# First layer by Strassen's seven products on three 768-token tiles, in a kernel of windowed attention and two MLPs

## The reference

```
c: chunk of 32 queries; its keys are 8 memory keys + 16 before + 32 + 8 after     (8 heads of 64)
x = softmax(q k^T / 8) v                          # 3072 x 512
h = max(x @ w1, x @ w2, x @ w3);  y = h @ w_out   # MLP 1: 512 -> 768 (three times) -> 512
u = y @ w_in2                                     # MLP 2: 512 -> 2048
g = u if u >= 1, 0 if u <= -1, else (u + 1)^2 / 4
out = g @ w_out2                                  # 2048 -> 512
```

## Time and profile before

| | |
|---|---|
| median of 3 runs | 984.15 us (984.12 to 984.52) |
| the profiled execution | 983.69 us |
| its span, first to last instruction | 981.6 us |
| TensorE busy | 968.8 us |
| VectorE, ScalarE, GpSimd busy | 469.6, 354.5, 150.0 us |
| moved by DMA | 181.52 MB, mean 185 GB/s |

### The profile page before, as it was taken

The page is one execution under the profiler, slowest core; times in us unless marked ns, Lnnn a source line. Parts: engine busy times, 40 slices in busy tenths (PEclk is TensorE's granted clock), DMA queues, the critical chain, the costliest instruction groups (busy, mean ns, idle before and its releaser), DMA issues.

```text
span 981.6 us, 18566 instructions
## 1 busy us (share of the span) xinstructions
PE 968.8 (99%) x7968; PEld 905.1 (92%) x7968; DVE 469.6 (48%) x713; ACT 354.5 (36%) x553; POOL 150.0 (15%) x176
## 2 busy tenths in 40 slices
PE   6999999999999999999999999999999999999998
PEld 5999999999999999999998888988888888888887
DVE  4662524244252434425456655566545666454452
ACT  3342212222222222222353625545354544444253
POOL 2022442405235230000000000000000000000000
PEclk9999999999999999999999999999999999999999
DMA  9462753645465361042735566655756545575532
GB/s 363 186 234 70 267 183 128 252 144 188 162 236 183 153 231 61 1 172 65 269 131 217 203 220 215 204 196 200 249 191 236 192 161 196 187 258 170 198 118 108
DMA packets 32206, 181.52 MB, mean 185 GB/s; under 512 B 3456, under 2 KB 7552, under 8 KB 21888
## 3 DMA queue, kind: packets, MB, share of 16 engines
q0 software_dynamic: 9216, 92.28, 27.0%
q1 hardware_dynamic: 22912, 88.09, 24.4%
HBM read 144.70 MB, written 35.65 MB: 184 GB/s over the span
## 4 chain that ended last, share of the span: by engine, by line
PE 98%; DMA 1%; DVE 0%; ACT 0%; issue 0%; SPq 0%
PE mlp_ps L491 23%; PE mlp_ps L492 23%; PE mlp_ps L493 23%; PE attn_ps L493 3%; PE scores_ps L493 3%; PE attn_ps L492 3%; PE scores_ps L492 3%; PE attn_ps L491 3%; PE scores_ps L491 3%; PE attn_ps L484 3%; PE scores_ps L457 2%; PE trans_ps L493 2%; PE trans_ps L492 2%; PE trans_ps L491 1%; PE trans_ps L466 1%; DMA qk_raw<-qk_l 1%
## 5 line engine op out<-in xcount | busy, mean ns | idle before, releaser
L491 PE MATMUL mlp_ps<-x_hi,w_hi 128*128 128x384 f32 x572 | 195.1, 341 | 0.0
L493 PE MATMUL mlp_ps<-x_lo,w_hi 128*128 128x384 f32 x572 | 191.5, 335 | 0.0
L492 PE MATMUL mlp_ps<-x_hi,w_lo 128*128 128x384 f32 x572 | 191.2, 334 | 0.0
L492 PE MATMUL mlp_ps<-yc,wi 128*128 128x384 f32 x448 | 150.7, 336 | 0.0
L493 PE MATMUL mlp_ps<-yc,wi 128*128 128x384 f32 x448 | 149.6, 334 | 0.0
L491 PE MATMUL mlp_ps<-yc,wi 128*128 128x384 f32 x448 | 149.6, 334 | 0.0
L787 ACT ACTIVATE ramp<-up,half_col 128x768 f32<-128x768 f32 x64 | 60.1, 939 | 197.4 <-DVE up L1004 178.2
L491 PEld LDWEIGHTS mlp_ps<-x_hi,w_hi 128*128 128x128 f32 x572 | 107.4, 188 | 1.9
L492 PEld LDWEIGHTS mlp_ps<-x_hi,w_lo 128*128 128x128 f32 x572 | 107.5, 188 | 0.0
L493 PEld LDWEIGHTS mlp_ps<-x_lo,w_hi 128*128 128x128 f32 x572 | 107.4, 188 | 0.0
L492 PEld LDWEIGHTS mlp_ps<-yc,wi 128*128 128x128 f32 x448 | 84.1, 188 | 8.8
(11 more groups left out here) (138 smaller groups left out, 1653.0 us busy)
## 6 DMA issues: line engine op xcount, KB each, us to landing
wi<-wi_scratch POOLq DMA_DIRECT2D x32, 1792.0 KB, 7.5
wo<-wo_scratch POOLq DMA_DIRECT2D x32, 1024.0 KB, 5.1
qk_raw<-qk_l SPq DMA_DIRECT2D x24, 768.0 KB, 8.1
wi_scratch<-stage_a SPq DMA_DIRECT2D x8, 1792.0 KB, 8.2
v_raw<-v_l SPq DMA_DIRECT2D x24, 512.0 KB, 4.8
wo_scratch<-stage_a SPq DMA_DIRECT2D x8, 1024.0 KB, 6.6
y_scratch<-y_stage SPq DMA_DIRECT2D x32, 192.0 KB, 2.6
y_raw<-y_scratch SPq DMA_DIRECT2D x8, 768.0 KB, 5.3
```

Of the source, the lines that this page charges most:

```text
L491: pe.matmul(out_ap, a_hi, b_hi, start=first, stop=False, skip_group_check=beside)
L492: pe.matmul(out_ap, a_lo, b_hi, start=False, stop=False, skip_group_check=beside)
L493: return pe.matmul(out_ap, a_hi, b_lo, start=False, stop=last, skip_group_check=beside)
```

## The change

MLP 1 keeps two tiles of 384 tokens (`first_tile`, `second_tile`; the second carries six groups of attention). The other 2304 tokens go through three tiles of 768 (`strassen_tile`, v = 0, 1, 2). In each, the six column blocks and three matrices make nine pairs of column blocks (`PAIRS_S = 9`), 27 in all, and each is made with seven products over 2 x 2 blocks, in a form with partial sums that are added up in PSUM: products 0, 2, 4 and 6 use one bank without clearing it, 3 and 5 another. ScalarE copies the bank after products 0, 2, 3 and 4 (`snapshot`), VectorE adds products 1 and 5 and the copy of 3 (`block_sum`), and takes the maximum over the three matrices (`block_max`). Attention of the next tile, six groups, is spread over the 63 product slots, one group in ten slots; tile 2 has none. Layer 2 of a tile is eight products (`l2_product`).

The left operands are made by GpSimd: an item is a pair, made in two halves (`split_half`), stored to `wi_scratch` by GpSimd's own queue and streamed back for each pair with `load_wi` into two buffers. There are 17 items (9 of MLP 1, 8 of MLP 2). Fourteen halves (`AHEAD`) are made during the two plain tiles, the first five (`EARLY`) with one staging buffer and the rest with two; the others are made one per pair. The right operands `yc1` are made from `x_raw` at each tile's start (`xc_sum`, `xc_high`, `xc_low`). `load_wi(0)` waits for the end of the second tile's layer 1.

MLP 2 uses the same scheme of products: five copies by ScalarE and three folds by VectorE in a period. Its output weights are no longer stored split; GpSimd loads them raw each period (512 KB for 1024) and splits them (`split_wo`).

```diff
-PRODUCTS = (("m1", 0, P, 4), ("m2", 3 * P, 2 * P, 5), ("m5", 2 * P, 2 * P, 6), ("m3", 10 * P, P, 1),
-            ("m4", 12 * P, P, 0), ("m7", 8 * P, P, 3), ("m6", 6 * P, P, 2))
+PAIRS_S = 3 * KFP
+EARLY, AHEAD = 5, 14
+PRODUCTS = ((W_A11, Y_B11), (W_A12, Y_B21), (W_S2, Y_T2), (W_S1, Y_T1), (W_S3, Y_T3), (W_S4, Y_B22), (W_A22, Y_T4))
...
# GpSimd
+            def split_half(n):
+                raw = w_raw[:, n % 2]
+                sums, both = staging(n)
...
+                pool.wait_ge(raw_in[n % 2], 16 * (n // 2 + 1))
...
+                pool.tensor_tensor(s3, a11, a21, ALU.subtract).then_inc(w_sums_done, 1)
+                pool.tensor_tensor(s1, a21, a22, ALU.add).then_inc(w_sums_done, 1)
+                pool.tensor_tensor(s2, s1, a11, ALU.subtract).then_inc(w_sums_done, 1)
+                pool.tensor_tensor(s4, a12, s2, ALU.subtract).then_inc(w_sums_done, 1)
+                if n >= EARLY + 2:
+                    pool.wait_ge(w_stored[n % 2], 16 * (n // 2))
+                elif 0 < n < EARLY:
+                    pool.wait_ge(w_stored[(n - 1) % 2], 16 * ((n - 1) // 2 + 1))
+                pool.tensor_copy(hi[:, 0:4 * P], raw).then_inc(w_hi_done, 1)
+                pool.tensor_copy(hi[:, 4 * P:7 * P], sums).then_inc(w_hi_done, 1)
+                pool.tensor_tensor(lo[:, 0:4 * P], raw, hi[:, 0:4 * P].bitcast(F32), ALU.subtract).then_inc(w_split, 1)
+                pool.tensor_tensor(lo[:, 4 * P:7 * P], sums, hi[:, 4 * P:7 * P].bitcast(F32), ALU.subtract).then_inc(w_split, 1)
...
+                pool.dma_start(wi_scratch[n // 2][:, n % 2 * W_COLS:(n % 2 + 1) * W_COLS], both).then_inc(w_stored[n % 2], 16)
+                if n + 2 < 2 * ITEMS:
+                    load_raw(n + 2)
...
+            load_raw(0)
+            load_raw(1)
+            for n in range(AHEAD):
+                split_half(n)
+            pool.wait_ge(mlp_done, TG + L1G)
+            load_wi(0)
+            load_wi(1)
+            for g in range(PERIODS_S):
+                if AHEAD + g < 2 * ITEMS:
+                    split_half(AHEAD + g)
+                pool.wait_ge(l1_done, 7 * (g + 1))
+                load_wi(g + 2)
...
+            for g in range(PERIODS):
+                split_wo(g)
+                if g + 1 < PERIODS:
+                    pool.wait_ge(wo_split, 2 * (g + 1))
+                    load_wo(g + 1)
+                if g + 2 < PERIODS:
+                    pool.wait_ge(prod_done, 7 * (g + 1))
+                    load_wi(PERIODS_S + g + 2)
# TensorE
+            def l1_product(g, i):
+                v, q = divmod(g, PAIRS_S)
+                if i == 0:
+                    pe.wait_ge(wi_in[g % 2], 16 * (g // 2 + 1))
+                    if q == 0:
+                        pe.wait_ge(x_split, 8 * (v + 1))
+                if i < 2 and q == 0:
+                    pe.wait_ge(y_copied, y_before(v) - 1 + i)
+                elif i < 2:
+                    pe.wait_ge(summed, 3 * g - 2 + 2 * i)
+                elif i == 3:
+                    if q and (q - 1) % 3:
+                        pe.wait_ge(merged, merges(g - 1) + 4)
+                    elif q:
+                        pe.wait_ge(c21_copied, (g - 1) // 3 + 1)
+                else:
+                    pe.wait_ge(snapped, 4 * g + (0, 0, 1, 0, 2, 3, 4)[i])
+                wcols, ycols = (slice(n * c, (n + 1) * c) for n, c in zip(PRODUCTS[i], (P, TT)))
+                w, x = wi[g % 2], yc1
+                begins = i in (0, 1, 3)
+                for j in range(2):
+                    last = three(l1_bank(g, i), (w[:, j, 0, wcols], w[:, j, 1, wcols], x[:, j, 0, ycols], x[:, j, 1, ycols]),
+                                 begins and j == 0, j == 1, not begins)
+                last.then_inc(l1_done, 1)
# ScalarE
+            def snapshot(g, i):
+                act.wait_ge(l1_done, 7 * g + i + 1)
...
+                copy(snap[:, f, t], l1_bank(g, i)).then_inc(snapped, 1)
# VectorE
+                dve.tensor_tensor(to[:, f, t], snap[:, f, t], other, ALU.add).then_inc(summed, 1)
...
+                dve.tensor_tensor(h_run[:, f, t], h_run[:, f, t], other, ALU.max).then_inc(merged, 1)
...
+            def xc_low(v, j, k):
+                dve.wait_ge(xc_hi_done, 4 * (2 * v + j) + HI_ORDER.index(k) + 1)
+                hi, lo = (yc1[:, j, i, Y_PARTS[k]] for i in range(2))
+                dve.tensor_tensor(lo, xc_source(j, k), hi.bitcast(F32), ALU.subtract).then_inc(x_split, 1)
```

More of the change, by code:

```diff
@@ L517, in layer1 @@
                 for k in range(KD):
-                    if ahead is not None and k == KD - 1:
+                    if ahead is not None and k == at:
                         ahead()
@@ L564, in tile_a @@
-                    layer1(t, a, f, 1)
-                    layer1(t, a, f, 2, ahead if attention and r else None)
-                if attention:
-                    weighted_v(n0 + GPT - 1, GPT - 1)
-                if t < TILES - 1:
-                    for d in range(KD):
-                        layer2(t, a, d)
+                    if r:
+                        transposes(n0 + j, (n0 + j) % 2)
+                    layer1(0, 0, f, 1)
+                    layer1(0, 0, f, 2, ahead if r else None)
@@ new lines, in second_tile @@
+            def second_tile():
+                for f in range(KF1):
+                    n = GT + f
+                    if f:
+                        h_high(1, f - 1)
+                        x_copy(n - 1)
+                    exponent(n, n % 2)
+                    h_first(1, 1, f)
+                    transposed(n)
+                h_high(1, KF1 - 1)
+                x_copy(2 * GT - 1)
+                xc_high(0, 0, 1)
+                xc_high(0, 0, 0)
+                xc_high(0, 0, 2)
+                y_out(1, 0)
+                xc_high(0, 0, 3)
+                xc_high(0, 1, 1)
+                y_out(1, 1)
+                xc_high(0, 1, 0)
+                xc_high(0, 1, 2)
+                xc_high(0, 1, 3)
+                y_out(1, 2)
+                y_out(1, 3)
@@ L745, in _, with yc_high @@
             w_high(1)
[L746 to L751 removed]
+            first_tile(range(A_FIRST, A_PIECES))
+            second_tile()
+            def yc_high(v, j, parts):
                 if v >= 2:
@@ new lines, in _, with fold @@
+            for v in range(TILES_S):
+                strassen_tile(v)
+                if v + 1 < TILES_S:
+                    xc_work(v + 1)
+            def fold(g, f, t):
+                c = up[:, g % 2, f, t]
+                if f:
+                    dve.wait_ge(copied, 5 * g + 4)
+                    m = m5[:, :]
+                else:
+                    i = (1, 5)[t]
+                    dve.wait_ge(prod_done, 7 * g + i + 1)
+                    dve.wait_ge(copied, 5 * g + 1 + t)
+                    m = prod[(g + i) % 2]
+                dve.tensor_tensor(c, c, m, ALU.add).then_inc(folded, 1)
```

885 lines of the change are left out of this document (577 added, 308 removed).

## The result

The changed kernel takes **1018.25 us** (median of 4 runs, 1016.66 to 1023.19) beside 984.13 for the kernel before in the same session: a ratio of 1.0356, 95% interval 1.032 to 1.0392. It is slower by 34 us. The forecast was 974.5, the range 957 to 992: wrong in sign and outside the range.

A forecast was written before the change was run, and what follows sets the result against it. TensorE, busy 968.8 of 981.6 us, was taken as the bound. Fewer matmuls (-28.1), stream (+12), xc (+3.5) and chain (+3) sum to -9.6, giving 974.5 us; range 957 to 992.

The forecast's parts named there:

- 162 matmuls fewer: Layer 1 of MLP 1: 1296 matmuls become 1134, at 0.1733 us each, -28.1 us.
- chain inside a pair, copies and folds: MLP 1 pairs: ScalarE copies between accumulating products have 0.24 us spare; 3 us lost over 27 periods, bounds 0 and 20.
- MLP 2: Period stays at 15.6 us with TensorE full; extra copies, folds and wo splitting cost 0.
- GpSimd ahead of the first Strassen tile: Fourteen halves end at 139, wi lands near 148 against layer 2's end at 147.3: at most 1 us late.
- xc at that boundary: Before the first Strassen tile, VectorE makes xc while GpSimd splits, sharing the SBUF lock: 3.5 us once, between 0 and 8.
- stream, tiles 0, 1, 2: Late wi loads in the Strassen tiles at 410 GB/s: 5, 3 and 4 us, sum 12, ends 0 and 26.
- pace of 0.32 behind waits: Matmuls falling to 0.32 us apart after waits; judged unlikely, since gaps of 1 us in 9 should not do that.
- the 0.06 of the rest: Leftover chance 0.06: both kinds of waits adding up past 990, or matmuls falling to the slower pace after waits.
- Rival B: Strassen tiles' stream: mixed loads and stores get 364 GB/s, costing 25.7 us in place of 12: 988 us, chance 0.17.
- rival C: Copies inside a pair become the bound: ScalarE 0.44 late each, TensorE loses 21.6 us: 986 us, chance 0.12.
- what would show it: Signs: 18 us more idle on wi, 10.5 and 7.5 us pairs, 8 to 11 landings, copy waits under 5, xc gap near 147.
- I am wrong if: Two conditions: wi landings stay at 7.5 us (stream hides, chance 0.20), or copies end the waits (chance 0.12).

The follow-up runs named there:

- run 8: Run 5 with wi loads from pair 2 of MLP 1 on cut from 1792 KB to 16 KB (no stream): 964.06 us, 0.9802 of the kernel before.
- run 11: Changed kernel, late start kept, with wi loads from pair 2 of MLP 1 on cut to 16 KB: 989.5 us, 1.0051 of the kernel before.
- run 1: Changed kernel with the first two wi loads issued behind split half 11 instead of 13: 1008.97 us, 1.026 of the kernel before.
- run 5: Changed kernel with split halves moved: twelve ahead, one per pair, three and two under layer 2 behind tiles 0 and 1: 998.04 us, 1.0132 of the kernel before.
- run 6: Run 5 with each wi load in two DMAs, the second waited for at product 2, in both MLPs: 982.93 us, 0.9996 of the kernel before.
- run 9: Run 6 with the first piece of wi issued after product 3 of the pair that frees the buffer: 975.77 us, 0.992 of the kernel before.
- run 10: Run 9 with the first piece of wi issued ahead of the split half's store instead of behind it: 982.69 us, 0.999 of the kernel before.
- run 4: Changed kernel making only the fourteen halves ahead and streaming those seven items repeatedly: 997.07 us, 1.0123 of the kernel before.
- run 3: Changed kernel loading only slivers of q, k and v for attention groups from 15 on: 1008.05 us, 1.026 of the kernel before.

## Why the prediction was wrong

**The accounts.** The changed kernel stands 54.2 us over run 8 (55.8 in the spans). TensorE's waits on wi are 34.8 more (37.0 - 2.2), on ScalarE 4.3 more (5.9 - 1.6), the lower clock takes 13.7: 52.8. Runs 11 and 8 share it out: 25.4 for the late start and the late last store, 28.8 for the stream beside its neighbours. Run 8 stands 8.0 above 956.1, and TensorE's waits make 7.6 of that: 2.2 on wi, 0.8 on copies in the tiles, 2.2 where MLP 2 begins (0.79, 0.96 and 0.47), 0.5 ahead of it and 1.9 in the first 27 us.

| step of the prediction | predicted | measured |
|---|---|---|
| 162 matmuls fewer | -28.1 | TensorE's busy time in run 8: 968.8 to 940.3, -28.5 |
| chain inside a pair, copies and folds | +3 | 0.8 of waits in run 8 |
| MLP 2 | 0 | period 15.64 as before, 2.2 at its start |
| GpSimd ahead of the first Strassen tile | at most +1 | wait of 18.07; 19.7 by run 11 against run 8 |
| xc at that boundary | +3.5 | 1.5 to 2.5 where wi is in time (runs 1, 5, 6, 9, 10); in the changed kernel it hides under the 18.07 |
| stream, tiles 0, 1, 2 | 5, 3, 4 | 14.6, 10.0, 4.1 (waits of 9.2, 6.2, 2.8, the rest mostly the clock) |
| the last tile's start | not seen | 4.24 on ScalarE; 6.8 by run 11 against run 8 |
| pace of 0.32 behind waits | in the 0.06 of the rest | 13.7 lost |

**The step that failed most is GpSimd's schedule** ("five early halves ... 10 us each, to 76; nine more at 6.9 end at 139"). It put the first load of wi at 139; it was issued at 156.56. The schedule had no spare, and each of its three parts ran over. The early halves ended at 85, not 76: the first raw load took 6.8 us (first sum at 33.67), and the stores were issued at 41.14, 52.63, 67.78, 76.00 and 84.45, since the third cast waited 6.75 for a store that took 10.5 us and not 6. The next seven took 7.4 each and not 6.9, 3.2 us in all (the seventh was stored at 135.95). Then VectorE's xc held GpSimd: sums of 128 columns took 1.06 us instead of 0.45, and two halves 10.2 and 9.3, 5.7 us in all. I had charged the lock to VectorE alone ("VectorE's h_lo ... took 1.49 us for 0.55", rows 10), at 3.5 us; the other side of it was GpSimd's, whose lateness was the bound at that moment. The Trainium skill ("SBUF — State Buffer", Who interferes with whom) says that such instructions exclude each other; the trace agrees, on both engines (1.06, and 1.49 in rows 10).

**The stream's mechanism was right, its size not.** Waits on wi at the first matmul of a pair, most where groups load, were foretold; the rate was taken as 410 GB/s, and tile 0 moved 349 at a DMA share of 0.95. Rival B named this (364 GB/s, 25.7 us in the stream). The stream cost 28.7 us in the three tiles, near the 25.7 of B, but that is in part luck: B had 12.3, 5.9 and 7.5 for 14.6, 10.0 and 4.1, and 9.4 of the measured cost came by the clock (half of 5.77 + 6.15 + 3.41 + 3.41 in tiles 0 and 1), which B did not have. B's 988 was still 30 us short, since it kept the forecast's start.

**The clock was dismissed** ("gaps of 1 us in 9 should not do that"). Inside the tiles gaps of 1 us did not; gaps of 2 to 5.2 us did. In runs 5 and 6 the clock turned 7.4 us of waits into 16.3.

**One wait was not seen.** By the kernel's text the staging of the halves lies where MLP 2's first yc0 goes, so yc_high(0), in ScalarE's queue ahead of the last tile's snapshots, waits for all 34 halves; the last store was issued at 422.90 and TensorE stood 4.24. Runs 4, 5 and 8, whose stores are done earlier, don't have it.

**Right were** the price of a matmul, the period of MLP 2, the spare time of the copies (rival C is out by run 8) and the order of the price of a late xc (3.5 charged, waits of 1.5 to 2.5 where wi is in time). **Of the signs** under "what would show it" only the 162 matmuls, the place of the waits and the 15.64 came as written. The idle time grew by 44.8 us, not 18. Pairs of tile 0 lasted 9.5 to 13.1 us, those of the last tile 7.3 to 8.6 and one 14.1. Landings of wi in the stage ran from 7.3 to 14.0 with a median of 9.1. Waits on copies came to 5.9, 4.24 of them behind yc_high. The gap near 147 did come, but DMA wi ended it, not xc. Neither condition of "I am wrong if" came true: they looked at the stream and the copies, and not at GpSimd's schedule.

What was won step by step: 20 us by the place of the halves in the queue (run 5), 22 more by the size and the time of the pieces of the load (runs 6 and 9). The change was sound in TensorE's terms and lost its gain to one queue that carried three kinds of work.

## What to carry to other kernels

A schedule of 14 steps in series that ends exactly when it is needed is late: add up its slowest rows, not its median ones, on both sides of every lock. Name a sign of being wrong for every part that has no spare, and not only for the one that worries you. When TensorE waits in lumps of some microseconds, read the granted clock beside the waits, in windows of the trace, and count only the work that falls into the low stretches. A streamed operand is best cut where its first reader needs it, so that each piece can be issued when its own part of the buffer is free: that was worth 22 us here with no byte less to move.

## What the runs showed of the hardware

- The granted clock of TensorE fell to 0.50 (1.2 of 2.4 GHz) at waits of 1.8 to 5 us between full-speed pairs, for 3.4 to 10.2 us, and came back to 1.00 each time. It did not at every such wait: it fell at waits of 2.00 (changed kernel), 1.99 (run 9) and 1.80 (run 4), and stayed up at 2.61 (run 6, 186.05) and 2.05 (run 3, 245.54). It also fell while TensorE stood for 18 us, and was back after 4.4 us of work.
- A load of wi of 1792 KB took 7.2 us at best and 9.6 to 12.6 in the crowded periods of tile 0; issued right behind another one it took 14.0 (15.8 in run 5); the DMA engines were 95% busy at 349 GB/s in tile 0, and had moved 417 to 422 in rows 8.
- A GpSimd sum of 128 columns took 0.45 to 0.47 us alone and 1.06 beside VectorE's two-input operations; both engines' streams slow down, and a half went from 6.9 us to 9.3 and 10.2.
